# Where expert 0's second weight load, x reads and first product stand, and expert 1's list and row requests

## The reference

```python
state = f[:, :, t, :, None] * state + einsum('bhd,bhe->bhde', k[:, :, t], v[:, :, t])
y[:, :, t] = einsum('bhd,bhde->bhe', q[:, :, t], state)
...
logits = x @ w_gate                       # 3072 x 8
for idx in argsort(-logits.flatten()):    # greedy, cap = 384 tokens for each expert
    ...
for e in range(E):
    h = maximum(x[mask] @ w1[e], 0.0)     # 384 -> 1024
    out[mask] = h @ w2[e]                 # 1024 -> 384
...
h = x @ w_in                              # 384 -> 2048
g = where(h > 0.0, h, exp(minimum(h, 0.0)) - 1.0)
out = g @ w_out                           # 2048 -> 384
```

## Time and profile before

| | |
|---|---|
| median of 3 runs | 856.01 us (855.54 to 856.14) |
| the profiled execution's own time | 854.62 us |
| its span | 852.7 us |
| PE busy | 790.8 us, 93% of the span |
| POOL, DVE, ACT busy | 528.3, 493.7, 465.6 us |
| mean granted TensorE clock | 0.978 |
| PE's share of the chain that ended last | 80% |

### The profile page before, as it was taken

The page is one execution under the profiler, slowest core; times in us unless marked ns, Lnnn a source line. Parts: engine busy times, 40 slices in busy tenths (PEclk is TensorE's granted clock), DMA queues, the critical chain, the costliest instruction groups (busy, mean ns, idle before and its releaser), DMA issues.

```text
span 852.7 us, 19225 instructions
## 1 busy us (share of the span) xinstructions
PE 790.8 (93%) x6378; PEld 748.9 (88%) x6378; DVE 493.7 (58%) x994; ACT 465.6 (55%) x980; POOL 528.3 (62%) x500
## 2 busy tenths in 40 slices
PE   3999995489999999999999999999999999999995
PEld 2888884378889899989988999899989999999995
DVE  6899998884784476448635764486448426430001
ACT  5677756142664277418732774187428744863653
POOL 8788884477784278527842785278518763964562
PEclk9999997599999999999999999999999999999999
DMA  7777690500410041004100410040004004100000
GB/s 194 208 207 205 195 366 35 184 2 2 148 30 8 23 149 29 13 17 150 28 10 25 148 29 11 19 150 28 20 10 153 25 29 148 28 2 29 1 1 28
DMA packets 33751, 65.83 MB, mean 77 GB/s; under 512 B 4560, under 2 KB 20944, under 8 KB 33280
## 3 DMA queue, kind: packets, MB, share of 16 engines
q1 hardware_dynamic: 27072, 50.36, 18.2%
q0 software_dynamic: 3136, 9.64, 3.5%
q10 hardware_dynamic: 3456, 4.72, 1.6%
HBM read 55.26 MB, written 9.44 MB: 76 GB/s over the span
## 4 chain that ended last, share of the span: by engine, by line
PE 80%; POOL 5%; issue 4%; DVE 4%; ACT 3%; DMA 1%; ACTq 0%; POOLq 0%; SPq 0%; DVEq 0%
PE o_ps L1420 8%; PE o_ps L1421 7%; PE o_ps L1422 7%; PE m_ps L1408 7%; PE m_ps L1409 6%; PE m_ps L1404 6%; PE m_ps L1360 4%; PE o_ps L1378 4%; PE m_ps L1358 4%; PE m_ps L1361 4%; PE o_ps L1380 3%; PE o_ps L1379 3%; PE a_ps L637 3%; PE y_ps L604 3%; PE r_ps L1277 2%
## 5 line engine op out<-in xcount | busy, mean ns | idle before, releaser
L1074 POOL TENSOR_TENSOR t_lo<-whole,t_hi 128x384 fp32r<-128x384 f32 x190 | 203.4, 1072 | 100.1 <-ACT t_hi L1155 98.4
L1102 POOL TENSOR_TENSOR whole<-whole,below 128x384 f32<-128x384 f32 x126 | 133.1, 1057 | 154.2 <-ACT below L1174 153.3
L1408 PE MATMUL m_ps<-y_hi,w_in_hi 128*128 128x384 f32 x384 | 134.4, 350 | 4.3 <-ACT y_hi L1186 4.3
L1420 PE MATMUL o_ps<-w_out_hi,t_hi 128*128 128x384 f32 x378 | 129.7, 343 | 3.4 <-POOL t_lo L1074 2.4
L1409 PE MATMUL m_ps<-y_hi,w_in_low 128*128 128x384 f32 x384 | 129.6, 338 | 0.0
L1421 PE MATMUL o_ps<-w_out_low,t_hi 128*128 128x384 f32 x378 | 127.5, 337 | 0.0
L1422 PE MATMUL o_ps<-w_out_hi,t_lo 128*128 128x384 f32 x378 | 127.1, 336 | 0.0
L1170 ACT ACTIVATE whole<-m_ps 128x384 f32<-128x384 f32 x128 | 62.8, 490 | 93.5 <-PE m_ps L1404 87.3
L1154 ACT ACTIVATE whole<-m_ps 128x384 f32<-128x384 f32 x64 | 31.5, 492 | 130.4 <-PE m_ps L1358 121.0
L1404 PE MATMUL m_ps<-y_lo,w_in_hi 128*128 128x384 f32 x384 | 87.0, 338 | 0.0
L1408 PEld LDWEIGHTS m_ps<-y_hi,w_in_hi 128*128 128x128 f32 x384 | 72.3, 188 | 6.4 <-issue 6.4
(11 more groups left out here) (236 smaller groups left out, 1690.7 us busy)
## 6 DMA issues: line engine op xcount, KB each, us to landing
w_raw<-w SPq DMA_DIRECT2D x16, 1536.0 KB, 7.8
f_in<-f_t SPq DMA_DIRECT2D x48, 96.0 KB, 2.5
k_in<-k_t SPq DMA_DIRECT2D x48, 96.0 KB, 2.6
q_in<-q_t SPq DMA_DIRECT2D x48, 96.0 KB, 2.5
v_in<-v_rows SPq DMA_DIRECT2D x24, 192.0 KB, 2.8
x_scratch<-x_row ACTq DMA_DIRECT2D x24, 192.0 KB, 2.5
w_in_raw<-w_in SPq DMA_DIRECT2D x1, 3072.0 KB, 11.6
w_out_raw<-w_out SPq DMA_DIRECT2D x1, 3072.0 KB, 20.8
```

The costliest lines, as they stand in the source:

```text
L1074: nc.gpsimd.tensor_tensor(t_lo[n % RING][:], whole[n % 3][:], t_hi[n % RING][:], ALU.subtract).then_inc(lo_made, 1)
L1102: nc.gpsimd.tensor_tensor(tile[:], tile[:], below[m % 2][:], ALU.subtract).then_inc(g_made, 1)
L1408: nc.tensor.matmul(bank[:], w_in_hi[:, t, cols], y_hi[:, t, :], start=(t == 0), stop=False)
L1420: nc.tensor.matmul(o_ps[t][:], hi[:, rows], w_out_hi[:, m, :], start=(m == 0), stop=False)
```

## The change

Six edits, all of them in expert 0:

1. SP waits for the second of expert 0's three row gathers to have landed (`gathered[TT - 2]`) before it issues w2's load.
2. ACT's three casts of w2 stand behind read_h(0), read_h(1), read_h(2) rather than ahead of the reads of x_hi.
3. PE's h0 waits for w1_low one piece at a time.
4. DVE does the first half of `compare_halves` ahead of the first piece of w2_low, the other half behind it.
5. Visit 0 stands behind y0 rather than h3, and visit 13 behind g9 rather than o5.
6. POOL issues expert 1's first gather at the head of m = 9 instead of its tail, and the second and third at the tails of m = 9 and 10 rather than 10 and 11; `rows_asked` follows the third.

```diff
-                visits = {("h", 3): 0, ("h", 4): 1, ("y", 2): 2, ("h", 6): 3, ("h", 7): 4, ("y", 4): 5, ("y", 6): 6, ("y", 7): 7,
-                          ("g", 2): 8, ("g", 3): 9, ("o", 1): 10, ("o", 2): 11, ("o", 3): 12, ("o", 5): 13}
+                visits = {("y", 0): 0, ("h", 4): 1, ("y", 2): 2, ("h", 6): 3, ("h", 7): 4, ("y", 4): 5, ("y", 6): 6, ("y", 7): 7,
+                          ("g", 2): 8, ("g", 3): 9, ("o", 1): 10, ("o", 2): 11, ("o", 3): 12, ("g", 9): 13}
...
+                else:
+                    sp.wait_ge(gathered[TT - 2], 16)
+                    sp.sem_inc(load_turn, 1)
                 sp.dma_start(w2_raw[:], w2[bass.ds(e, 1)].rearrange("a (k p) n -> p (a k) n", p=P)).then_inc(w2_loaded, 16)
...
+                ahead = 1 if start else 0
                 own = MI if routing else MI - HELPED
                 for m in range(own + 1):
+                    if start and m == gather_at:
+                        gather(k + 1, 1 - slot, 0)
...
-                    if routing and gather_at <= m < gather_at + TT:
-                        gather(k + 1, 1 - slot, m - gather_at)
-                        if m == gather_at + TT - 1:
+                    if routing and gather_at <= m < gather_at + TT - ahead:
+                        gather(k + 1, 1 - slot, m - gather_at + ahead)
+                        if m == gather_at + TT - ahead - 1:
                             pool.sem_inc(rows_asked, 1)
...
+                        if start and m < PIECES:
+                            raise_second(k, m)
...
-            for piece in range(PIECES):
-                raise_second(0, piece)
...
-                if m == 0:
+                if m == 0 and not start:
                     pe.wait_ge(w1_split, k * PIECES + PIECES)
...
+                        if m == 0 and start and not low:
+                            pe.wait_ge(w1_split, k * PIECES + (t + 1))
...
+            compare_half(0)
             lower_second(0, 0)
-            compare_halves()
+            compare_half(1)
             for piece in range(1, PIECES):
                 lower_second(0, piece)
```

More of the change, by code:

```diff
@@ L1522, in begin, with compare_half @@
                 begin_tiles(v, then, logits, consts, scan, slice(0, tiles), False)
+            def compare_half(half):
+                compare_first(v, consts, scan, slice(half * tiles // 2, (half + 1) * tiles // 2)).then_inc(hit_ready, 1)
             def compare_halves():
                 for half in range(2):
-                    compare_first(v, consts, scan, slice(half * tiles // 2, (half + 1) * tiles // 2)).then_inc(hit_ready, 1)
+                    compare_half(half)
             def search(r, slot, before_y=None, k=None, last=False):
```

## The result

The changed kernel takes 860.88 us (median of 16 runs, 856.62 to 862.89) beside 855.84 us of before. The ratio of all runs is 1.0044, 95% interval 1.0027 to 1.0060: slower by about 3.8 us (the medians differ by 5.0 us), where I forecast 3.8 us faster. The profiled execution takes 859.01 us with a span of 857.1 us, 4.4 us more than before.

A forecast was written before the change was run, and what follows sets the result against it. PE bounds the kernel, busy 93% of the span. Terms +0.6 - 1.3 - 1.5 - 2.1 + 0.5 = -3.8 us, so 850.8 us against the profiled 854.62 (852.2 on the median); range 850.4 to 855.2.

The forecast's parts named there:

- What is late next there: Expert 1's start: w1_low from about 245.0, x_lo or t_lo perhaps late for PE; +0.5 us, bounds 0 and 1.6.
- The turns: DVE and POOL at expert 0's start: strict turns, one instruction waits until the other engine's has ended; reached at 186.75.
- The start: Expert 0's start: first product 2.3 us earlier, but reached 1.2 us later and visit 2 at 192.7; +0.6 us.
- Rival B: Slow clock moves to expert 0's start, behind 187: +1.2 us, 853.4 us in all; chance 0.18 shared with another rival.
- Visit 13: Visit 13 behind nine products: PE's 1.28 us standstill for slot_hot goes, -1.3 us.
- the slow stretch near 234: Behind visit 13's standstill: 11 product steps at 0.32 instead of 0.175 us go, -1.5 us (0 to -1.5).
- x0: Expert 1's first rows: earlier gathers end PE's 2.07 us wait before x0, reached at 248.4; -2.1 us.
- A: Expert 0's start: w2 lands after 6.2 us, start -0.5, total -4.9 us, 851.1 us; chance 0.12.
- C: Slow stretch stays or moves (+1.5), POOL and DVE hold each other at 244 to 252 (+1.1): 854.8 us; chance 0.14.
- D: Expert 0's start: w2 late, slower overall if landing past 183.1; at 184, 858.6 us; chance 0.08.

The follow-up runs named there:

- e4_both_late: Kernel before with visit 13 behind g9 and expert 1's gathers earlier, no edit of the start; ratio to before 1.0038.
- e5_psum: Changed kernel with small operands of DVE's steps behind expert 1's list in PSUM, x0 also waiting for the first third of w1_low; ratio to before 0.9965.
- e1_start: Kernel before with only the start's edits (w2 load, w2 casts, h0, compare_halves, visit 0); ratio to before 1.0021.
- e9_w2_at_once: e7_psum_order with w2 issued right behind w1 instead of held back; ratio to before 0.9959.
- e6_order: Changed kernel with expert 0's compare_halves taken apart and put behind the first and second piece of expert 1's w2_low; ratio to before 0.9997.
- e7_psum_order: Changed kernel with both the PSUM operands of e5_psum and the moved comparison of e6_order; ratio to before 0.9971.
- e3_gathers: Kernel before with only expert 1's gathers and rows_asked moved earlier; ratio to before 0.9979.
- e11_before_psum: Kernel before with only the operands of DVE's small steps in PSUM and x0 waiting for the first third of w1_low; ratio to before 0.9988.
- e2_visit13: Kernel before with only visit 13 moved behind g9; ratio to before 1.0001.
- e8_late_mended: e7_psum_order with the start of the kernel before (start's edits undone); ratio to before 0.9969.
- e10_search_first: e7_psum_order with the second and third piece of expert 0's w2_low moved behind the search's first two comparisons; ratio to before 0.9939.
- e12_psum_search_first: e5_psum with the w2_low move of e10_search_first; ratio to before 0.9958.

## Why the prediction was wrong

**The step that failed** is the one under "What is late next there": w1_low of expert 1 "starts at about 245.0". I kept DVE's way from the list to the comparison at the length it had before, 6.4 us, and took turns with POOL into account only for the comparison and w1_low. It took 13.4 us, w1_low started at 252.8, and the term put at +0.5 us (0 to 1.6) came to a wait of 6.6 us and a slow stretch of 2.7 us. The terms of the sum then make +0.9 - 1.3 - 1.5 - 2.1 + 9.3 = +5.3 us; expert 1's first y_hi is 5.1 us later than before, and the span 4.4 us longer. I had moved visit 13 and let POOL follow PE, and did not ask what POOL's idle 2.73 us had been good for. Two experiments show it: e4_both_late has the wait without the start's edits, e5_psum takes it away without touching POOL.

**The turns** were half right. The one-by-one layout of the start held, since both engines had long instructions there and each reached the other's end. It does not hold against a stream: DVE waits for the rest of a gather, the subtraction and t_lo together, up to 2.6 us for a step of 0.17. The Trainium skill, SBUF — State Buffer, "Who interferes with whom", which I used only for the start, says that a DVE instruction with two SBUF inputs contends with a GpSimd instruction that reads SBUF, and that one with at most one SBUF input, outside its two-port modes, does not. The traces agree with both: the subtraction takes 2.12 us with two in the changed kernel and 0.17 us with one in e5_psum.

**The start.** Predicted +0.6 us with `reached` at 186.75 and visit 2 at 192.7; the profile has 186.25, 193.05 and +0.9 us at y_hi (+0.5 in e1_start). w2 took 7.4 us to land, for 7.7. Rival B came in as well: PE stood 1.7 us at visit 1 and the clock was at 1.2 GHz from 187 to 190.5. The mechanism was right, but B's price was not: y_hi comes 19.6 to 19.7 us behind `reached` in the four profiles with this slow stretch (the changed kernel, e1_start, e5_psum, e9_w2_at_once) and 18.8 us in the two without it (e6_order, e7_psum_order), so the stretch costs 0.8 us, not 1.2. With B as priced the start would have been +1.8.

**Visit 13, the slow stretch near 234, x0.** The wait is gone, the clock there stays at 1.00, x0 starts at 249.12 (forecast 248 to 249) without a wait. These gains came, -4.2 us at x0 with the start's +0.9 in them, and were lost at the next step, x1. One term was less sure than I had it: e3_gathers and e11_before_psum keep the wait before visit 13 and show no slow stretch behind it, so its 1.5 us belong to some executions of the kernel before, not to all.

**The other rivals.** A did not happen. C named the place, POOL and DVE at 244 to 252, at 1.1 us; it was the right mechanism at an eighth of its size (8.8 us more than forecast). D, w2 late, did not happen. That the slower side should come only through w2 was the second fault: my price of the contention was bounded by the instructions that I had seen contend, not by all with two SBUF inputs. The ends of the range were also added up 0.1 to 0.2 us off: by the terms given they are 850.6 and 855.3.

## What to carry to other kernels

Before you close a gap on the bounding engine, list who worked in the shadow of that gap: the engines behind it idle too, and a third may live on their pause. On this pair, count every DVE step with two SBUF inputs against POOL's stream, however small it is; one operand in PSUM frees it (7.0 us here). Where an in-order engine stops at the answers of another, shorten the way to the answer, not the way to the first product: 2.7 us at the first product gave nothing, 3.0 us at `reached` gave 1.8.

## What the runs showed of the hardware

A `tensor_scalar` of 24 numbers with one SBUF input also waited for POOL, 1.04 us in e5_psum, where it stands right behind the start of a t_lo:

```profile
234.53 1.04 DVE L1694 TENSOR_SCALAR open_tok<-own 128x24 f32<-128x24 f32 x1
```

POOL's t_lo there runs from 234.52 to 235.54, and the step ends at 235.57. Not every such step waits: in the changed kernel a `tensor_scalar` of 8 numbers (L1688) takes 0.17 us at 239.97, inside a gather. What decides stays open.

The first product comes 9.6 us behind the first gather in the profiles of before and e3_gathers, 10.1 and 10.0 in e2_visit13 and e8_late_mended, 8.1 and 7.7 in e4_both_late and e11_before_psum, all with the same start in the code. In the first four the first gather lands after 5.9 us, in the other two after 5.0 and 4.7, with both weight loads under way. The starts of these six run from 37.8 to 40.2 us, so a single profile of this start does not tell differences of 2 us. With w2 held back (edit 1) it is steadier: in the seven such profiles the first product comes 6.8 to 6.9 us behind the first gather. Among them the starts are 39.4 to 40.6 us, and 37.5 in e10_search_first and e12_psum_search_first, so the gain of 1.8 us stands clear of that spread and the +0.5 us of e1_start against before does not.

A standstill of 1.7 us at visit 1 was followed by the 1.2 GHz level in the changed kernel, e1_start, e5_psum and e9_w2_at_once, and not in e6_order and e7_psum_order. What decides between them stays open.
